# Attention, token and channel MLP, routed experts on one core: the opening of the attention worked in head pairs

## The reference

```python
q_s = softmax(q, axis=-1)                 # over the 64 numbers of a row
k_s = softmax(k, axis=2)                  # over the 576 rows
kv  = einsum('bhsd,bhse->bhde', k_s, v)
x   = einsum('bhsd,bhde->bhse', q_s, kv)  # heads side by side: 576 x 512
u   = x + (relu(x.T @ w_tok1) @ w_tok2).T
x1  = u + relu(u @ w_ch1) @ w_ch2
# then each row goes to one of 8 experts: p * relu(x1 @ w1[e]) @ w2[e]
```

## Time and profile before

| | us |
|---|---|
| median of 3 runs | 726.22 (726.21 to 726.36) |
| the profiled execution | 726.45 |
| its span (first to last instruction) | 724.3 |
| PE busy | 712.8 |
| DVE / ACT / POOL busy | 305.7 / 233.1 / 139.7 |
| first chunk of the channel MLP starts (us from the span's start) | 42.59 |

### The profile page before, as it was taken

One profiled execution on the slowest core, in us unless ns is written; L12 is line 12 of the kernel. 1 busy time (PEld: TensorE's weight loads), 2 busy tenths in 40 slices (PEclk: granted clock), 3 DMA queues, 4 the chain that ended last, 5 costly groups with the idle time before them and its releaser, 6 DMA issues.

```text
span 724.3 us, 14261 instructions
## 1 busy us (share of the span) xinstructions
PE 712.8 (98%) x4970; PEld 647.7 (89%) x4971; DVE 305.7 (42%) x641; ACT 233.1 (32%) x453; POOL 139.7 (19%) x168
## 2 busy tenths in 40 slices
PE   7999999999999999999999999999999999999997
PEld 6799999999999999999999999788888888888885
DVE  5776232235232235232225722785445552221631
ACT  3673142023142023142021133321536542222621
POOL 6565020002020002020000015022221322121311
PEclk9999999999999999999999999999999999999999
DMA  9952131012131012100010340114744561010100
GB/s 239 358 113 67 34 99 33 1 35 67 33 99 33 1 35 67 33 33 1 1 39 1 117 165 15 53 44 135 282 160 147 185 227 58 23 56 25 35 21 12
DMA packets 71997, 57.65 MB, mean 80 GB/s; under 512 B 54892, under 2 KB 57228, under 8 KB 71952
## 3 DMA queue, kind: packets, MB, share of 16 engines
q1 hardware_dynamic: 68432, 47.58, 22.0%
q0 software_dynamic: 3520, 9.44, 3.9%
HBM read 48.79 MB, written 10.31 MB: 82 GB/s over the span
## 4 chain that ended last, share of the span: by engine, by line
PE 96%; DVE 1%; POOL 1%; DMA 1%; issue 0%; ACT 0%; SPq 0%; POOLq 0%; DVEq 0%
PE bank L644 43%; PE bank L792 16%; PE bank L817 16%; PE bank L573 5%; PE bank L607 3%; PE bank L804 3%; PE bank L599 2%; PE bank L675 2%; PE bank L729 1%; PE bank L543 1%; PE bank L560 1%; PE bank L584 1%; POOL qb L1815 1%; PE bank L652 1%; DMA qraw<-in_q_dram 1%; DVE wc_l L1549 0%
## 5 line engine op out<-in xcount | busy, mean ns | idle before, releaser
L644 PE MATMUL bank<-u_h,wc_h 128*128 128x288 f32 x384 | 117.3, 306 | 0.1
L644 PE MATMUL bank<-hid_h,wc_h 128*128 128x288 f32 x384 | 115.0, 300 | 0.0
L644 PE MATMUL bank<-hid_l,wc_h 128*128 128x288 f32 x384 | 113.2, 295 | 0.0
L644 PE MATMUL bank<-u_h,wc_l 128*128 128x288 f32 x384 | 113.1, 295 | 0.0
L644 PE MATMUL bank<-u_l,wc_h 128*128 128x288 f32 x384 | 113.1, 294 | 0.0
L644 PE MATMUL bank<-hid_h,wc_l 128*128 128x288 f32 x384 | 113.0, 294 | 0.0
L792 PE MATMUL bank<-wslots,xgT_h 128*128 (+1 forms) x344 | 110.6, 402 | 0.0
L817 PE MATMUL bank<-wslots,hT_h 128*128 (+1 forms) x336 | 104.2, 391 | 0.0
L1498 DVE SCALAR_TENSOR_TENSOR hid_l<-bank,hid_h 128x288 fp32r<-128x288 f32 x96 | 43.2, 454 | 107.7 <-ACT hid_h L998 107.0
L998 ACT ACTIVATE hid_h<-bank 128x288 fp32r<-128x288 f32 x96 | 39.2, 409 | 112.0 <-PE bank L644 111.6
L817 PEld LDWEIGHTS bank<-wslots,hT_h 128*128 128x128 f32 x336 | 62.6, 188 | 13.4 <-DVE hT_l L1712 0.5
(11 more groups left out here) (270 smaller groups left out, 1053.7 us busy)
## 6 DMA issues: line engine op xcount, KB each, us to landing
w1raw<-in_moe_w_dram SPq DMA_DIRECT2D x20, 512.0 KB, 5.3
w2raw<-in_moe_w_dram SPq DMA_DIRECT2D x20, 512.0 KB, 5.0
wc_raw<-in_moe_w_ch_dram SPq DMA_DIRECT2D x8, 768.0 KB, 10.2
vb<-in_v_dram SPq DMA_DIRECT2D x32, 128.0 KB, 3.1
x_rows<-x1n SPq DMA_DIRECT2D x16, 256.0 KB, 2.3
kb<-in_k_dram SPq DMA_DIRECT2D x24, 128.0 KB, 3.0
qb<-in_q_dram SPq DMA_DIRECT2D x24, 128.0 KB, 2.9
qraw<-in_q_dram SPq DMA_DIRECT2D x2, 512.0 KB, 5.6
```

Of the source, the lines that this page charges most:

```text
L644: last = pe.matmul(to, lhsT, rhs, start=(m == 0), stop=(m == len(mms) - 1))
```

## The change

- The parts of the q softmax are head pairs (`PAIRS`: heads 0-1 and 2-3, all five layers) where they were layers. This holds for maxima, subtraction, exponent, sum, inverse and scaling, in all batches. `mixed` and `qT_tiles` wait per pair.
- q of the first group is loaded in three pieces: pair 0, the last layer of all heads, pair 1 (own semaphore `q_second`). The next loads stand in the order k of group 0, `wt1`, q of group 1, k of group 1 (before: k 0, k 1, `wt1`, q 1).
- The opening has another order on PE, ACT and DVE, with 94 + 16 `keep_warm` products (before: 84 + 14 + 16).
- POOL makes the high parts of `wc1` j = 0 and 1 (before: 0; ACT made 1). ACT and DVE split other pieces of `wc2` at other places.

```diff
@@ loads on SP
-            load_raw(qraw, q, 0, 0, q_first[0])
+            load_pair(0, q_first[0])
+            sp.dma_start(qraw[0:REST, 0, :, TOP, :], q[0, 0:HG, FULL:S, :].rearrange("h p d -> p h d")).then_inc(q_first[0], 16)
+            load_pair(1, q_second)
             load_raw(kraw, k, 0, 0, k_first[0])
-            load_raw(kraw, k, 1, 0, k_first[1])
             sp.dma_start(wt1[:, 0:TOP, :], ...)
             sp.dma_start(wt1[0:REST, TOP, :], w_tok1[FULL:S, :]).then_inc(tok_w_in, 16)
             load_raw(qraw, q, 1, 0, q_first[1])
+            load_raw(kraw, k, 1, 0, k_first[1])
@@ PE
             def qT_tiles(n, g, tiles, bn, later):
                 for j in tiles:
-                    if j < 2:
-                        pe.wait_ge(qn_done, 2 * n + j + 1)
+                    pe.wait_ge(qn_done, 2 * n + j // 2 + 1)
@@ mixed
                 for c in columns:
+                    pe.wait_ge(qn_done, 2 * n + c + 1)
                     for i in range(NI):
-                        if c == 0 and i in (IHALF[0].start, IHALF[1].start):
-                            pe.wait_ge(qn_done, 2 * n + 1 + int(i > 0))
@@ PE, opening
-            keep_warm(84)
+            keep_warm(94)
+            mixed(0, 0, (0,))
             steps(("mT", 0))
-            keep_warm(14)
+            mixed(0, 0, (1,))
             steps(("ksub", 0))
+            qT_tiles(0, 0, (0, 1), None, False)
             keep_warm(16)
-            mixed(0, 0, (0,))
-            qT_tiles(0, 0, (0, 1), None, False)
-            mixed(0, 0, (1,))
-            steps(("mT", 1), ("kv", 0), ("ksub", 1))
+            mixed(1, 1, (0,))
             qT_tiles(0, 0, (2, 3), None, False)
-            mixed(1, 1, (0,))
+            steps(("kv", 0), ("mT", 1), ("qT01", 1), ("ksub", 1))
+            mixed(1, 1, (1,))
             steps(("h1", 0))
-            qT_tiles(1, 1, (0, 1), None, True)
-            mixed(1, 1, (1,))
             qT_tiles(1, 1, (2,), None, True)
             steps(("kv", 1))
             qT_tiles(1, 1, (3,), None, True)
@@ ACT, opening
-            steps(0, "qexp", "qexp2", "kexp", "kexp2", "qT01")
+            steps(0, "qexp", "qexp2")
             steps(1, "qexp")
             steps(0, "mix")
-            steps(1, "qexp2", "kexp")
-            steps(0, "qT23")
-            steps(1, "kexp2")
-            split_token_weights(0)
+            steps(1, "qexp2")
+            steps(0, "qT01", "kexp", "kexp2", "qT23")
+            for m in range(KT):
+                split_token_weights(m)
+            steps(1, "qT01", "kexp", "kexp2")
             steps(0, "h1")
-            split_token_weights(1)
-            qT_out(1, 1, (0, 1))
             steps(1, "mix")
             qT_out(1, 1, (2,))
-            split_half(1, 0)
+            split_half(2, 0)
             qT_out(1, 1, (3,))
+            split_half(2, 1)
             for j in range(2 * KD):
                 u_out(0, 0, j, first=True)
                 if j == 0:
-                    split_half(1, 1)
                     steps(1, "h1")
                 elif j < 3:
-                    split_half(2, j - 1)
-                elif j < 5:
-                    split_half(3, j - 3)
+                    split_half(3, j - 1)
                 else:
-                    split_second(j - 5)
+                    split_second(j - 3)
@@ DVE, opening
-            steps(0, "qmax", "qmax2", "qrec", "kmax", "kmax2")
-            first_qsum(0, 1)
+            steps(0, "qmax", "qmax2")
+            for part in range(2):
+                first_qsum(0, part)
+                first_qrec(0, part)
+            steps(0, "kmax", "kmax2")
+            steps(1, "qmax")
             steps(0, "mT")
-            first_qrec(0, 0)
-            steps(0, "ksub", "ksub2")
-            steps(1, "kmax", "qmax", "qmax2", "kmax2")
+            steps(1, "qmax2", "kmax")
             first_qsum(1, 0)
             first_qrec(1, 0)
-            steps(1, "mT")
+            steps(0, "ksub", "ksub2")
             first_qsum(1, 1)
             first_qrec(1, 1)
+            steps(1, "kmax2", "mT")
             steps(0, "kv")
             steps(1, "ksub", "ksub2")
             split_token_weights()
             steps(0, "h1")
+            split_first(0, 0)
             steps(1, "kv")
-            for half in range(2):
-                split_first(0, half)
+            split_first(0, 1)
             for j in range(2 * KD):
                 u_out(0, j)
                 if j == 0:
                     steps(1, "h1")
-                if j in (2, 3):
-                    split_first(2, j - 2)
-                if j == 6:
-                    split_second(0)
+                if j in (1, 2):
+                    split_first(2, j - 1)
+                if j in (4, 6):
+                    split_second(j - 4)
@@ POOL
             for n in range(NG):
                 softmax_steps(n)
-            pool.wait_ge(wc1_in[0], 16)
-            for half in range(2):
-                part = slice(half * CH // 2, (half + 1) * CH // 2)
-                pool.tensor_copy(wc1[0][:, 0, part], wc1_raw[:, 0, part]).then_inc(wc1_hi_pool, 1)
+            for j in range(2):
+                pool.wait_ge(wc1_in[j], 16)
+                for half in range(2):
+                    part = slice(half * CH // 2, (half + 1) * CH // 2)
+                    pool.tensor_copy(wc1[0][:, j, part], wc1_raw[:, j, part]).then_inc(wc1_hi_pool, 1)
             for j in (1, 3):
...
                     pool.tensor_tensor(wc1[1][:, j, part], wc1_raw[:, j, part], wc1[0][:, j, part], ALU.subtract).then_inc(wc1_lo_pool, 1)
```

More of the change, by code:

```diff
@@ L254, in build @@
         k_first, q_first = ([sem(f"{x}_first{n}") for n in range(NG)] for x in "kq")
+        q_second = sem("q_second")
         k_in, q_in, v_in = sem("k_in"), sem("q_in"), [sem(f"v_in{g}") for g in range(NG)]
@@ L319, in build @@
         IHALF = (slice(0, 2), slice(2, NI))
+        PAIRS = tuple(slice(c * (HG // CG), (c + 1) * (HG // CG)) for c in range(CG))
         BLOCKS = ((0, P), (P, P), (2 * P, REST // 2))
@@ L421, in load_unit, with load_pair @@
                     sp.dma_start(w2raw[:, c:c + 2, :], e2[:, c:c + 2, :]).then_inc(raw_in[i], 16)
+            def load_pair(c, landed):
+                pair = q[0, PAIRS[c], 0:FULL, :]
+                sp.dma_start(qraw[:, 0, PAIRS[c], 0:TOP, :].rearrange("p h i d -> p h (i d)"),
+                             pair.rearrange("h (p i) d -> p h (i d)", p=P)).then_inc(landed, 16)
             for buffer_free in x1_stored:
@@ L920, in qexp @@
                 act.wait_ge(qsub_done, 2 * n + part + 1)
-                x = queries(n)[:, IHALF[part], :].rearrange("p i n -> p (i n)")
+                x = queries(n)[:, :, part * P:(part + 1) * P]
                 act.activation(x, x, ACT.Exp).then_inc(qexp_done, 1)
@@ L1002, in batch @@
                     chunk_out(b, idx)
-                    if first and idx < 2 * HEAD:
-                        split_second(KC - 2 * HEAD + idx)
+                    if first and idx == HEAD:
+                        split_second(KC - 1)
                     if not more and idx == NCB - NC2:
@@ L1224, in qmax_of @@
                         dve.wait_ge(q_in, 16 * (HG + 1) * (n - NG + 1))
-                if n == 0 and part == 1:
+                if n == 0:
                     dve.wait_ge(padded, 1)
-                dve.tensor_reduce(qmax[g][:, IHALF[part], :], loaded(n, qraw, qb)[:, IHALF[part], :, :], AX_X, ALU.max).then_inc(qmax_done, 1)
+                    if part == 1:
+                        dve.wait_ge(q_second, 16)
+                dve.tensor_reduce(qmax[g][:, :, PAIRS[part]], loaded(n, qraw, qb)[:, :, PAIRS[part], :], AX_X, ALU.max).then_inc(qmax_done, 1)
             def qsum_of(n, g, part):
                 dve.wait_ge(qexp_done, 2 * n + part + 1)
-                return dve.tensor_reduce(qsum[g][:, IHALF[part], :], by_head(queries(n))[:, IHALF[part], :, :], AX_X, ALU.add)
+                return dve.tensor_reduce(qsum[g][:, :, PAIRS[part]], by_head(queries(n))[:, :, PAIRS[part], :], AX_X, ALU.add)
             def qden_of(g, these, steps_before):
                 dve.wait_ge(qrec_step, steps_before + 1)
-                dve.tensor_scalar(qden[g][:, these, :], qsum[g][:, these, :], 1e-9, None, ALU.add).then_inc(qrec_step, 1)
+                dve.tensor_scalar(qden[g][:, :, these], qsum[g][:, :, these], 1e-9, None, ALU.add).then_inc(qrec_step, 1)
                 dve.wait_ge(qrec_step, steps_before + 2)
-                dve.reciprocal(qrec[g][:, these, :], qden[g][:, these, :]).then_inc(qrec_step, 1)
+                dve.reciprocal(qrec[g][:, :, these], qden[g][:, :, these]).then_inc(qrec_step, 1)
             def qrec_of(n, g, part):
@@ L1244, in qrec_of @@
                     done.then_inc(qrec_step, 1)
-                    qden_of(g, slice(0, NI), 3 * (n + int(n >= NG)))
+                    qden_of(g, slice(0, HG), 3 * (n + NG))
             def first_qsum(n, part):
@@ L1250, in first_qrec @@
             def first_qrec(n, part):
```

(32 more changed lines are left out.)

2 lines of the change are left out of this document (1 added, 1 removed).

## The result

| | median of runs | range |
|---|---|---|
| before | 726.39 us | 726.21 to 726.47 (6 runs) |
| changed | 729.49 us | 729.05 to 731.64 (6 runs) |

The medians differ by 3.1 us. The ratio, taken over the runs and not over the two medians, is 1.0046, 95% interval 1.0036 to 1.0057: slower by 0.46%. The forecast was 728.6, range 725.0 to 730.0. The changed kernel spreads over ten times the range of the old one (2.6 us against 0.26), and its profiled execution is its slowest (731.64, span 729.6).

The account below looks back on a forecast made before the run. The prediction took the opening's chain (load, maxima, POOL, ACT, sums, POOL) before the first mixed as the bound. A first chunk later by 2.4 gave 726.45 + 2.4 = 728.85, less 0.23 for the median: 728.6 us, range 725.0 to 730.0.

Parts of the forecast that it names:

- Opening without the clock: From start to first chunk: chunk at 45.4 or 44.6 against 42.59, plus 2.8 or 2.0 us; plus 2.4 taken.
- the stand: Inside u_tile 0, PE does two kvd products, then waits for low h1, from 29.4 to 32.5.
- Casts hold DVE: At the token weights, POOL's casts block DVE's four subtractions; plus 2.4 us with this, minus 0.5 without.
- Second collision: At tiles 1 and 2, split_first(2, .) takes turns with POOL's subtraction, making tile 5 late: cost 1.15 us.
- Other edits at nothing: split_half(1, .) off ACT, the extra q load, moved wc2 parts and keep_warm in the opening priced at 0.
- What happens after 42.59 should keep its length: The stream after the first chunk stays as long as before, priced at 0; a changed length would mean wrong.
- Rival 3: PE idles so long before tile 0 that its granted clock falls: another 1.5 to 2 us, 730.7; chance 0.06.
- The collision: At the token weights, DVE's four pieces alternate with POOL's casts and subtractions; low h1 ends 32.45 against 30.02.

Follow-up runs that it names:

- c1: The changed kernel run again unedited, first later group: five runs, median 728.93 us, ratio 1.004; its profiled execution took 727.72.
- e1: The changed kernel, but POOL waits until DVE has split the token weights before its casts of wc1 j = 1: 724.96 us, ratio 0.9979.
- e8: The changed kernel with one wait: POOL starts the low part of wc1 j = 3 after DVE's four wc1 pieces: 728.22 us, ratio 1.0014.
- c2: The changed kernel run again unedited, second later group, for one profile: 728.67 us.
- e5: e1 plus a second wait: POOL starts the low part of wc1 j = 3 after DVE's four wc1 pieces: 723.86 us, ratio 0.9966.
- e6: The kernel before, with the q softmax of batches 1 to 3 in head pairs instead of layers, opening untouched: 725.61 us, ratio 0.9989.
- e4: The changed kernel with all splits of wc1 and wc2 on the engines and tiles of the kernel before: 727.63 us, ratio 1.0008.
- e9: e5 with PE made to wait idle before u_tile 0 until DVE has done split_first(0, 1): 727.99 us.
- e2: The kernel before, with the casts of wc1 j = 1 given to POOL and taken off ACT: 728.37 us, ratio 1.0027.

## Why the prediction was nearly right

- **Opening without the clock, +2.8 or +2.0: right, at the upper end.** c1 shows +2.7, the first chunk at 45.28 for 45.4, step by step: `mixed` at 10.99 (10.65), DVE at the token weights at 26.22 (25.95), low `h1` ended 32.28 (32.45), `h1` of group 1 at 34.19 (34.35), tile 1 at 35.15 (35.25), tile 2 at 36.42 (36.5), tile 5 at 41.32 (41.55). PE's arrival at tile 0 was off, 29.50 for 28.95; it hid in the stand.
- **Casts hold DVE: right**, which no row of before showed. In the profile after, the two second casts took 2.05 instead of 1.59 together and DVE's pieces beside them 1.28 and 0.84; e1 took all of it away. The prediction set a rule of the Trainium skill, SBUF — State Buffer, section Who interferes with whom, beside its rows; the trace agrees with it.
- **Second collision, 1.15: right in place**, 0.9 as a wait and, taken away, 0.86 in the first chunk (e8 against c2) and 1.1 in the median (e5 against e1).
- **Other edits at nothing: held in c1, not quite in the profile after.** There `wt1` landed at about 11.2 (10.0) and q 1 at 13.3 (12.0). PE waited for neither, but DVE's maxima waited 0.59 for q 1, and `mixed` of group 1 began at 19.99, in c1 at 18.74. It hid in the stand of tile 0. Whether the added load or the spread of landings did it isn't shown.
- **"What happens after 42.59 should keep its length": wrong**, the term priced at 0 measures -1.2 to -1.4 in the changed kernel, one of the prediction's own signs of being wrong. The reason given, that a pair is ready no later than a layer part, was true but priced at nothing: the second half is smaller and is ready earlier. e6 shows 0.9 of it; the other 0.4 isn't traced.
- **Rival 3, the clock, at 0.06: much too low.** It fell in two of three profiles and, by the mean clock, in at least 10 of the 12 runs. The stand was forecast right, and the price of a fall (1.5 to 2) nearly so; how likely it was in such a stand was not. In the profile after, the first chunk is 3.8 later than in c1: 1.86 because low `h1` began 1.86 later, as much as POOL's casts, which waited for the loads of the weights (25.49 against 23.63); the other 2.0 came with half clock. In c2 it is 1.3: 0.56 and 0.74.

So that the forecast of +2.4 came so near the measured +3.1 is in part luck, two errors that nearly cancel: +2.7 - 1.3 = +1.4, which is c1's profiled execution (+1.27), and the clock with the later landings brings most executions to 3. The collision, the mechanism that the forecast named, was right. Why landings vary by 1.9 us stays open.

## What to carry to other kernels

When work is moved to GpSimd, write down which DVE instructions with two SBUF inputs will run beside it, and price each turn as a full instruction of the other engine, however small the waiting one is: here 64 columns, 0.22 alone, took 1.82. If DVE is on the critical path, let POOL wait on a semaphore for DVE's last urgent piece: two such waits took this change from 0.46% slower to 0.34% faster. A stand of PE can have a second price behind it, the clock: here half clock came with stands of 2.2 to 3.1 us in five profiles, at a price of 0.7 to 2.0 us where it could be compared, and filler products ahead of the wait saved it.

## What was unexpected of the hardware

- Where both DVE and POOL had such work queued, the profiles show them alternate, one instruction each: in c1 and after, four DVE pieces worth 1.5 us took 5.5 and 6.0 us.
- The granted clock fell during an idle stand of PE, or within 1 us behind it, at stands of 2.16 us (c2), 2.48 (e8), 2.66 (e4), 2.74 (after) and 3.13 (e9), and did not at 2.15 (c1) and 1.99 (e2). It stayed at half for 3.4 us in c2, e4, e8 and e9, and for 6.8 (33.35 to 40.18) in the profile after. The length alone does not decide it: two of the 11 runs of e9 show a mean clock of 1.000.
- A wait of 0.27 us in front of three weight loads of the stream went away when 1280 numbers were cut into 640 and 640 instead of 512 and 768: the side engines' latency counted although they are idle more than half of the time.
